# Linear attention ahead of two expert layers: first round finished at once, state on VectorE, loads chained to landings, last round in other banks

## The reference, cut to what matters

```python
# q, k, v: batch 4, heads 8, sequence 768, head size 64, float32
gamma = 1.0 - 2.0 ** (-5.0 - np.arange(H))
for t in range(S):
    state = gamma * state + einsum('bhd,bhe->bhde', k[:, :, t], v[:, :, t])
    y[:, :, t] = scale * einsum('bhd,bhde->bhe', q[:, :, t], state)
# y as x of shape (3072, 512), then
x = ((x @ w_a) * (x @ w_b)) @ w_out            # first feed-forward, d_ff 1536
# then top-1 of 8 experts for each row: relu(x @ w1[e]) @ w2[e], times two gates
```

## Time and profile before

| | before |
|---|---|
| median of 3 runs | 1066.01 us (1065.79 to 1068.99) |
| the profiled execution | 1067.78 us, its span 1066.0 us |
| PE busy | 1042.6 us, 98% of the span |
| DVE, ACT, POOL busy | 407.7, 293.4, 110.8 us |
| first matmul of the first feed-forward starts | 87.62 us |

### The profile page before, as it was taken

How to read it: one execution, slowest core, us unless ns; L and a number is a source line. 1 busy time by engine, 2 the same in 40 slices (tenths; PEclk the granted TensorE clock), 3 DMA queues, 4 the chain that set the end, 5 groups by cost and what they waited for, 6 DMA issues and landing times.

```text
span 1066.0 us, 18259 instructions
## 1 busy us (share of the span) xinstructions
PE 1042.6 (98%) x6489; PEld 932.6 (87%) x6490; DVE 407.7 (38%) x800; ACT 293.4 (28%) x550; POOL 110.8 (10%) x108
## 2 busy tenths in 40 slices
PE   6999999999999999999999999999899999999997
PEld 5888999999999999999999999998688888888886
DVE  3445432222223223223223212458445445354542
ACT  2444332212112112122122121331334334243431
POOL 4770000000000000000000000000121111111111
PEclk9999999999999999999999999999999999999999
DMA  9997801001001001001001002200744433335311
GB/s 364 363 336 224 200 1 61 1 1 60 1 1 60 1 1 60 1 1 60 1 20 41 1 30 79 79 21 32 276 144 146 176 116 118 115 132 198 115 35 35
DMA packets 34091, 98.69 MB, mean 93 GB/s; under 512 B 4397, under 2 KB 10797, under 8 KB 34032
## 3 DMA queue, kind: packets, MB, share of 16 engines
q1 hardware_dynamic: 28976, 83.17, 23.1%
q0 software_dynamic: 4480, 13.90, 3.8%
q10 hardware_dynamic: 576, 0.79, 0.2%
HBM read 80.54 MB, written 18.09 MB: 93 GB/s over the span
## 4 chain that ended last, share of the span: by engine, by line
PE 94%; DMA 4%; DVE 1%; issue 1%; ACT 0%; POOL 0%; ACTq 0%; DVEq 0%; POOLq 0%
PE bank L952 38%; PE bank L970 19%; PE bank L1310 13%; PE bank L1287 13%; PE bank L1295 2%; PE bank L580 2%; DMA rows<-in_steps 2%; PE bank L633 1%; PE bank L531 1%; DMA xg<-x_dram,idx_gather 1%; PE bank L545 1%; PE bank L753 1%; PE bank L566 1%; DMA qdec_t<-in_consts 1%; PE bank L762 1%
## 5 line engine op out<-in xcount | busy, mean ns | idle before, releaser
L952 PE MATMUL bank<-x_hi,wab_hi 128*128 128x384 f32 x768 | 258.6, 337 | 0.0
L952 PE MATMUL bank<-x_hi,wab_lo 128*128 128x384 f32 x768 | 258.2, 336 | 0.0
L952 PE MATMUL bank<-x_lo,wab_hi 128*128 128x384 f32 x768 | 257.6, 335 | 0.0
L896 DVE TENSOR_TENSOR g_sb<-bank,b_sb 128x384 f32<-128x384 f32 x96 | 53.5, 557 | 368.6 <-PE bank L952 368.6
L952 PEld LDWEIGHTS bank<-x_hi,wab_hi 128*128 128x128 f32 x768 | 144.7, 188 | 3.9 <-issue 0.2
L952 PEld LDWEIGHTS bank<-x_lo,wab_hi 128*128 128x128 f32 x768 | 144.5, 188 | 3.7
L952 PEld LDWEIGHTS bank<-x_hi,wab_lo 128*128 128x128 f32 x768 | 144.4, 188 | 0.0
L1287 PE MATMUL bank<-w,xe_hi 128*128 (+1 forms) x432 | 136.2, 397 | 1.2 <-DVE xe_lo L642 1.1
L712 ACT COPY b_sb<-bank 128x384 f32<-128x384 f32 x96 | 46.3, 482 | 255.3 <-PE bank L952 255.3
L970 PE MATMUL bank<-wo_hi,g_hi 128*128 128x512 f32 x288 | 116.0, 403 | 0.0
L970 PE MATMUL bank<-wo_hi,g_lo 128*128 128x512 f32 x288 | 113.7, 395 | 0.0
(11 more groups left out here) (161 smaller groups left out, 1114.3 us busy)
## 6 DMA issues: line engine op xcount, KB each, us to landing
raw<-in_w SPq DMA_DIRECT2D x64, 512.0 KB, 4.8
rows<-in_steps SPq DMA_DIRECT2D x20, 768.0 KB, 7.8
rows<-in_steps SPq DMA_DIRECT2D x24, 256.0 KB, 7.3
wab_raw<-in_weights SPq DMA_DIRECT2D x24, 256.0 KB, 7.7
x_dram<-y_sb SPq DMA_DIRECT2D x8, 768.0 KB, 4.0
xT_dram<-x_all SPq DMA_DIRECT2D x6, 768.0 KB, 11.9
x_raw<-xT_dram SPq DMA_DIRECT2D x6, 768.0 KB, 5.3
wo_raw<-in_weights SPq DMA_DIRECT2D x4, 768.0 KB, 10.0
```

What stands on the lines that cost most here:

```text
L896: nc.vector.tensor_tensor(g_sb[:, f % 2], bank[2 * (f % 2)][:, 0:GT], b_sb[:, f % 2], ALU.mult).then_inc(g_done, 1)
L952: ins = nc.tensor.matmul(bank[to][:, 0:GT], wab(w, f, j), x[s][:, k, :], start=(k == 0 and m == 0), stop=(k == KD - 1 and m == 2))
```

## The change

- **Round 0.** PE finishes round 0 (within of step 0, cross and within of step 1) ahead of scores(1).
- **State.** `state_dec` and its ACT instructions go; DVE runs four SCALAR_TENSOR_TENSOR of 128x64 for a step, (old state x decay) + kv. kv of the two steps of a round lie in banks 6 and 7, and `kv_done` counts steps.
- **Loads.** Steps 0 and 1 come as halves (q, k for scores; then k, v). Every later transfer is issued when an older one has landed. v of a round is split: the second step's v waits for a landing of q and k. The tables come after round 5's issues. v of steps 22 and 23 stand ahead of `load_wo(0)`, which waits for `load_wab(0)` to land; the two stores of x wait for `load_wo(0)`.
- **Last round.** cross and within of round 11 write banks 2 and 3, and wait for the probabilities of step 23 instead of the eviction of round 10. `up` of f = 1 waits for the last eviction.
- **Other moves.** POOL's second group of x_lo stands behind all decays; DVE's first weight split stands behind the last round's work; kdec_t is ACT's first transfer, and POOL waits for qdec_t only ahead of its first q_dec.

```diff
@@ sp_attention
-        for r in range(RB):
-            for i in range(ROUND):
-                load_qk(r, i)
-                load_v(r, i)
-        sp.dma_start(ident, ...)            (and rt, gates)
-        for r in range(ROUNDS - RB):
-            sp.wait_ge(kv_done, r + 1)
-            sp.wait_ge(q_dec_done, q_decs_until(r))
-            for i in range(ROUND):
-                load_qk(r + RB, i)
-            if r > 0:
-                sp.wait_ge(attn_done, r + CREDIT)
-                for i in range(ROUND):
-                    load_v(r - 1 + RB, i)
+        def landed(kind_in, n):
+            sp.wait_ge(kind_in[n % CH], (n // CH + 1) * 16)
+
+        def load_ahead(n):
+            if n < 2 * ROUND:
+                landed(qk_in if n == ROUND else v_in, 1 if n == ROUND else 0)
+            else:
+                landed(v_in, n - 2)
+            load_qk(n // ROUND, n % ROUND)
+            landed(v_in if n == ROUND else qk_in, n - 1)
+            load_v(n // ROUND, n % ROUND)
+
+        for i in range(ROUND):
+            sp.dma_start(rows[:, i, 0:2], steps_in[i][:, 0:2]).then_inc(qk_in[i], 16)
+        sp.dma_start(rows[:, 0, 2:4], steps_in[0][:, 2:4]).then_inc(v_in[0], 16)
+        landed(qk_in, 0)
+        sp.dma_start(rows[:, 1, 2:4], steps_in[1][:, 2:4]).then_inc(v_in[1], 16)
+        for n in range(ROUND, CH):
+            load_ahead(n)
+        for r in range(ROUNDS - RB):
+            n = ROUND * (r + RB)
+            sp.wait_ge(kv_done, states_until(r // RB, r % RB))
+            sp.wait_ge(q_dec_done, q_decs_until(r))
+            landed(qk_in, n - 2)
+            load_qk(r + RB, 0)
+            landed(qk_in, n - 1)
+            load_qk(r + RB, 1)
+            if r != 1:
+                done = max(r, 1)
+                sp.wait_ge(attn_done, done + CREDIT)
+                load_v(done - 1 + RB, 0)
+                landed(qk_in, n)
+                load_v(done - 1 + RB, 1)
+            if r == 2 * RB - 1:
+                sp.dma_start(ident, ...)    (and rt, gates)
         load_wab(sp, 0)
-        load_wo(sp, 0)
         sp.wait_ge(attn_done, ROUNDS - RB + CREDIT)
         for i in range(ROUND):
             load_v(ROUNDS - 1, i)
+        sp.wait_ge(wab_in[0], 4 * 16)
+        load_wo(sp, 0)
+        sp.wait_ge(wo_in[0], 16)
         sp.wait_ge(attn_read, (READY + 2) * TG // ROUND + CREDIT)
         store_x(sp, 2)
@@ pool_attention
-                if b == 2 and j < READY:
-                    split_ready_lo(pool, j)
+                if b == 2 and j == 0:
+                    split_ready_lo(pool, 0)
+        split_ready_lo(pool, 1)
@@ dve_attention, new_states and the loop
-                dve.wait_ge(state_dec_done, b * (CH - 2) + c)
-                nc.vector.tensor_tensor(states[:, c], state_dec, kv, ALU.add).then_inc(state_new, 1)
+                dve.wait_ge(state_new, b * (CH - 1) + c)
+                for p in range(PAIRS):
+                    ins = nc.vector.scalar_tensor_tensor(states[:, c, p], states[:, c - 1, p], kdec_t[:, H + p:H + p + 1], kv[:, p],
+                                                         ALU.mult, ALU.add)
+                ins.then_inc(state_new, 1)
...
-                if (b, j) == (B - 1, RB - 1):
-                    split_wab_lo(dve, 0)
                 probabilities(b, j)
@@ pe_attention
+        def output(b, j):
+            if round_no(b, j) == ROUNDS - 1:
+                pe.wait_ge(probs_done, STEPS)
+            else:
+                pe.wait_ge(attn_read, round_no(b, j) + CREDIT)
+            opened = []
+            if (b, j) == (0, 0):
+                within(b, j, 0, opened)
+                cross(b, j, 1, opened)
+                within(b, j, 1, opened)
+                return
...
@@ pe_ff, up
+                if f == 1:
+                    pe.wait_ge(attn_read, ROUNDS + CREDIT)
```

More of the change, by code:

```diff
@@ L446, in evict @@
                 ins = nc.scalar.copy(x_all[:, at_n:at_n + ROUND, o::2],
-                                     bank[4 + o].rearrange("p (i a t) -> p i a t", i=ROUND, a=PAIRS // 2))
+                                     bank[out_bank(b * RB + j) + o].rearrange("p (i a t) -> p i a t", i=ROUND, a=PAIRS // 2))
             ins.then_inc(attn_read, 1)
[L450 to L456, removed]
-                    ins = nc.scalar.activation(state_dec[:, p], states[:, c - 1, p], ACT.Copy, scale=kdec_t[:, H + p:H + p + 1])
-                ins.then_inc(state_dec_done, 1)
+        act.dma_start(kdec_t, const_in[:, C_KDEC:C_QDEC]).then_inc(kdec_in, 16)
         for o in range(2):
@@ L571, in within @@
-        def within(b, j):
-            for i in range(ROUND):
-                c = ROUND * j + i
-                pe.wait_ge(probs_done, b * CH + c + 1)
-                if i not in kv_steps(j):
-                    pe.wait_ge(v_in[c], (b + 1) * 16)
-                for a in range(0, PAIRS, 2):
-                    for p, o in ((a, 0), (a + 1, 0), (a, 1), (a + 1, 1)):
-                        h = 2 * p + o
-                        ins = nc.tensor.matmul(out_at(i, p, o), rows[:, c, 3, h * D:(h + 1) * D], probs[j][:, i, h, :],
-                                               start=False, stop=(i == ROUND - 1 and p >= PAIRS - 2), skip_group_check=True)
-            ins.then_inc(attn_done, 1)
+            return bank[out_bank(r) + o][c0:c0 + D, (i * (PAIRS // 2) + p // 2) * P:(i * (PAIRS // 2) + p // 2 + 1) * P]
@@ new lines, in cross @@
+        def cross(b, j, i, opened):
+            c = ROUND * j + i
+            pe.wait_ge(q_dec_done, b * (CH - 1) + c)
+            pe.wait_ge(state_new, b * (CH - 1) + c)
+            pe.sem_inc(cross_ready, 1)
+            q_at = (ROUND * round_no(b, j) + i) % (2 * ROUND)
+            for a in range(0, PAIRS, 2):
+                for p, o in ((a, 0), (a + 1, 1), (a + 1, 0), (a, 1)):
+                    half_p, corner = slice(o * D, (o + 1) * D), (o, p % 2)
+                    ins = nc.tensor.matmul(out_at(round_no(b, j), i, p, o), states[half_p, c - 1, p, :], q_dec[half_p, q_at, p * P:(p + 1) * P],
+                                           start=corner not in opened, stop=False, skip_group_check=True)
+                    opened.append(corner)
+            if i == ROUND - 1:
+                ins.then_inc(cross_done, 1)
@@ new lines, in within @@
+        def within(b, j, i, opened):
+            c = ROUND * j + i
+            pe.wait_ge(probs_done, b * CH + c + 1)
+            if i not in kv_steps(j):
+                pe.wait_ge(v_in[c], (b + 1) * 16)
+            pe.sem_inc(cross_ready, 1)
+            for a in range(0, PAIRS, 2):
+                for p, o in ((a, 0), (a + 1, 0), (a, 1), (a + 1, 1)):
+                    h, corner = 2 * p + o, (o, p % 2)
+                    ins = nc.tensor.matmul(out_at(round_no(b, j), i, p, o), rows[:, c, 3, h * D:(h + 1) * D], probs[j][:, i, h, :],
+                                           start=corner not in opened, stop=(i == ROUND - 1 and p >= PAIRS - 2), skip_group_check=True)
+                    opened.append(corner)
+            if i == ROUND - 1:
+                ins.then_inc(attn_done, 1)
@@ L584, in pe_attention @@
         scores(0, 0)
         kv(0, 0)
-        for b in range(B):
-            for j in range(RB):
-                if (b, j) != (B - 1, RB - 1):
-                    scores(*following(b, j))
-                    kv(*following(b, j))
-                cross(b, j)
-                within(b, j)
+        output(0, 0)
+        scores(0, 1)
+        kv(0, 1)
+        for r in range(1, ROUNDS):
+            if r + 1 < ROUNDS:
+                scores((r + 1) // RB, (r + 1) % RB)
+                kv((r + 1) // RB, (r + 1) % RB)
+            output(r // RB, r % RB)
```

56 lines of the change are left out of this document (20 added, 36 removed).

## The result

The changed kernel takes 1079.15 us (1078.42 to 1081.33, 4 runs), the kernel before 1067.50 on the same chip (1065.79 to 1070.38, 4 runs): a ratio of 1.011 with a 95% interval of 1.008 to 1.014. It is slower by 11.65 us where 4.2 us faster was forecast. The span went from 1066.0 to 1077.3 us, by 11.3, and the first feed-forward matmul starts at 98.56 us instead of 87.62, 10.9 later. So nearly all of the loss lies in attention, as the forecast had placed the gain.

What follows compares the result with a forecast made beforehand. The prediction held bytes and matmuls nearly level in attention, with time lost at both ends. Lead 3.1, middle - 0.75 and end + 1.9 gave 4.25 us faster: median 1061.8 us, range 1058.6 to 1064.2.

Steps and rivals of the forecast that it cites:

- The chain: Loads issued on landings: 3.2 us without own bytes against 2.8 to 3.4 us of cover; on the edge, sum left unchanged.
- The page's 2.0 us: Fixed cost of a transfer by the Trainium skill; leaves 0.8 us of cover to spare and no bubble.
- bubbles in the chain: Rival, 8 rounds from kv(4) on: time without bytes costs 8(x - 0.35); at x = 1.5, 1071.0 us; chance 0.07.
- x: Per round, us without bytes beyond what is in flight; 0.4 allowed, 0.88 cancels the gain, over 1.28 means slower.
- The opening: Rounds 0 and 1: half loads and round 0 first; kv(0) ends near 12 instead of 14.5, scores(1) start at 15 to 17.
- lead: At kv(4), gated by v of step 9 landing at 34.9: it ends at 35.5 instead of 38.6, 3.1 us earlier.
- The middle: From v of step 11 to v of step 19: at 0.36 MB/us it gives back 0.75 us, bounds 0 and 3.1.
- bytes take it back: Rival: transfers stay at 0.329 MB/us from 41 us on, lead 0.15 at step 19, 1064.0 us; chance 0.2.
- State on VectorE: Four DVE instructions a step, 0.87 us (bounds 0.6 and 1.67), cost and gain on the path 0.
- The end: From 69.73 us to the feed-forward: eviction wait of 1.26 us goes, v earlier; gives 1.9 us, bounds 0.6 and 4.0.

Runs made afterwards that it cites:

- d1: c2 with q and k of step n issued when those of step n-3, not n-2, have landed, from step 3 on; v free: 1067.65 us, ratio 0.9991.
- e3: The kernel after with the waits on landings taken away for steps 0 to 5 alone: 1075.25 us, ratio 1.0065.
- d3: The kernel before with round 0 finished first, without the increment in within: 1067.92 us, ratio 0.9991.
- c2: The kernel after with no wait on a landing and without the increment in within: 1065.88 us, ratio 0.9973.
- d2: c2 without the increments ahead of kv and cross as well: 1064.29 us, ratio 0.9953.
- b1: The kernel before with the state on VectorE alone (kv in two banks): 1068.61 us, ratio 1.0000.
- c4: The kernel before with the last round in banks 2 and 3, without the increment in within: 1067.54 us, ratio 0.9988.
- e1: The kernel after with no wait on a landing, the order of the issues kept: 1070.48 us, ratio 1.0015.
- c3: The kernel after, chain included, without the increment in within: 1078.80 us, ratio 1.0099.
- c1: The kernel before with only the increment of cross_ready added in within: 1072.34 us, ratio 1.0040.
- b2: The kernel before with round 0 finished first, with the increment in within: 1073.24 us, ratio 1.0047.
- b3: The kernel before with the last round in banks 2 and 3, with the increment in within: 1071.86 us, ratio 1.0030.
- f2: The kernel before without its increments ahead of kv and cross: 1067.23 us, ratio 0.9995.
- f1: d4 without any of the increments (within, kv and cross): 1062.34 us, ratio 0.9935.
- d4: c2 with v of steps 22 and 23 ahead of load_wab(0): 1063.63 us, ratio 0.9957.

## Why the prediction was wrong, point by point

- **The chain (the step that failed).** The prediction set 3.2 us that are no bytes of the transfer's own against 1.05 to 1.3 MB, "2.8 to 3.4 us of cover", called it "on the edge" and let the 0.379 MB/us of an unchained queue stand. It counted all that had been issued as bytes still to come, though q and k of step n-1 had been on their way for some time (2.6 us where step 6 lands). The sum to make is bytes in flight over the whole issue-to-landing time. In the kernel after, q and k of a step (768 KB, steps 2 to 10) took 5.6 to 6.9 us, 6.1 in the mean; two at a time are 2 x 0.786 / 6.1 = 0.26 MB/us, and with v, a third as much again, 0.34 as an estimate. The profile has 300 to 320 GB/s (0.30 to 0.32 MB/us) from 10 to 40 us, against 376 to 403 before. So v of step 5 landed at 25.4 us, not 20.4, 5.0 late. v of step 9 stands behind this pace and behind the landing of q and k of step 10, was issued at 40.1 us and landed at 45.9 instead of 34.9, 11.0 late. kv(4) ended at 47.15 instead of 35.5. With three steps of q and k in flight and v free (d1) the loss is gone.
- **The page's 2.0 us.** The Trainium skill (DMA: Bandwidth & Descriptors, Anatomy of one DMA) has 2.0 us fixed, in a fit for transfers that GpSimd issues, which by the estimate left cover to spare. No run here has a transfer alone, so its fixed part is not shown. The least that a transfer in the chain took is 3.4 us, for 256 KB (v of step 2), of which 0.7 are bytes at 0.379 MB/us. The 3.2 us of the prediction are no measure of it either: other loads were issued behind that first one from 1.2 us on, before it had landed at 6.0.
- **The rival "bubbles in the chain"** (0.07) is what happened, though its formula falls short. At 310 GB/s, the mean of 20 to 40 us, a round's 2.01 MB take 6.5 us, so x is 1.2, against the 0.4 that I had allowed and the 0.88 from which it decides. That gives 8 x (1.2 - 0.35) = 6.8 us, or 2.6 us slower than before, and x stays below the 1.28 that it wanted for a slower result; measured were 11.65 us. It covered the rounds from kv(4) on only; the opening lost as well (e3), and the half clock and the late v of step 9 came on top.
- **The opening.** scores(0) start at 5.66 (forecast 5.1), kv(0) ends at 13.8 (12), scores(1) start at 18.09 (15 to 17); round 0 alone is worth nothing (d3: 0.9991). Without chain and increment (c2) kv(4) ends at 37.5: a **lead of 1.1 us, not 3.1**. The prediction had PE there first and waiting for bytes; in c2 PE has no wait for v there, its own work is what is late. In d2, where PE does wait there (0.79 us), kv(4) ends at 36.9.
- **The middle.** In c2 the bytes of 40 to 60 us come at 354 GB/s and PE has no wait for them there; from 64 us on it waits 3.4 us for v. That is the rival "bytes take it back", late. 1.50 us of it, for step 22, go with the weights ahead of that v in the queue; the other 1.9, for steps 18 to 21, can't be theirs.
- **State on VectorE.** Four instructions in 0.86 us (forecast 0.87), and b1 gives 1.0000. Right. Each lasts 276 ns and starts about 195 after the one ahead.

```profile
13.87 0.86 DVE L514 SCALAR_TENSOR_TENSOR states<-states,kdec_t,bank 128x64 f32<-128x64 f32 x4 [1.46 <-PE bank L558]
```

- **The end.** The wait of 1.26 us for the eviction is gone in the kernel after; c4, the banks alone without the increment, has a ratio of 0.9988, 1.3 us, the size of that wait, though its interval reaches past 1. A new wait came behind: `up` of f = 2 waits for the split of the next weights. It isn't the chain's: e1, without one, waits 1.22 us there, and c3, with the chain and without the increment in `within`, not at all. All seven profiles with that increment have the wait (c1, which adds nothing else, 0.38 us), the other thirteen don't. Why was not shown.

```profile
109.92 0.41 PE L984 MATMUL bank<-x_hi,wab_hi 128*128 128x384 f32 x1 [0.68 <-DVE wab_lo L323]
```

- **The increment** was no step of the prediction. I took the new `within` for a move of code. It is 4.1 us in any version whose PE is not waiting already, the size of the whole gain that I had forecast: e1, the change without its chain, is not faster than before, and c2, the same without the line, is, by 0.27% (interval 0.08 to 0.46).
- **All together**: the chain costs 8.7 us of what is in e1; the increment costs e1 4.6; the rest is worth 2.9 us by the ratio of c2 to before (2.3 by the medians), with an interval of 0.9 to 4.9 us. The 4.25 that was forecast lies inside it; but by the opening's row it would be luck, since the lead was 1.1 us and not 3.1.

## What to carry to other kernels

Ahead of issuing a transfer on the landing of an older one, take the issue-to-landing time from the trace (here 5.6 to 6.9 us for 768 KB) and ask whether the bytes in flight over that time reach the rate at which the kernel eats them; if not, let one more be in flight before giving the order up. Read a diff of the busiest engine for instructions of their own that only signal, and count them with the moves. When idle time "for nothing" stands at regular distances in the records, look at the instruction packets before looking for a semaphore.

## What the runs showed of the hardware

- In the chain, 768 KB took 5.6 to 6.9 us from issue to landing, 2.1 us of it bytes at the unchained pace, and 256 KB of v took 3.4 to 6.5 (steps 2 to 7). The first 40 us moved 300 GB/s with two steps of q and k in flight, 360 with three and v free, 370 with no chain; with three, each q and k issued between 13.8 and 24.6 us took 7.0 to 8.2 us.
- PE stands idle now and then, in e1 every 122 to 124 matmul records, for 0.2 to 2.3 us (b2, b3); where a packet of 16 KB of instructions was looked for it goes on 2.2 to 2.9 us after it. That it waits for this piece of program is inferred from place and time. The increment in `within`, an instruction of its own, brings or lengthens this idle: 7.0 us of it in e1 and 7.1 in c1, 2.3 in the kernel before, which has such increments ahead of kv and cross alone. Without any there was none in d2 and f2 and 0.4 in f1; d4, without the one in `within`, had 3.0, so executions differ too.
- In the kernel after, after 3.43 and 2.63 us of idle the granted clock of a 10 us stretch (40 to 50 us) read 0.58, and 32 records took 3.68 us instead of 1.97.
